# The order of work between the last attention chunk and the feed-forward: logits in two goes, the row softmax moved back, half rows side by side, slot weights in two halves

## The reference, cut to what matters

```python
# x: 3072 tokens x 320, from a gated recurrent attention over 4 batches x 8 heads x 768 steps x 40
logits = x @ phi                              # 3072 x 32: 8 experts with 4 slots each
d = softmax(logits, axis=0)                   # over tokens: what goes into a slot
slot_input = (d.T @ x).reshape(8, 4, 320)
slot_out[e] = relu(slot_input[e] @ w1[e]) @ w2[e]        # 320 -> 1024 -> 320
c = softmax(logits, axis=1)                   # over slots: how a token is put together
x = c @ slot_out.reshape(32, 320)
out = relu(x @ w_in) ** 2 @ w_out             # 320 -> 2048 -> 320
```

## Time and profile before

| | |
|---|---|
| median of 3 runs | 392.47 us (391.86 to 392.49) |
| profiled execution | 392.09 us |
| its span, first to last instruction | 390.4 us |
| PE busy in the span | 371.8 us (95%) |
| DVE, ACT, POOL busy | 236.3, 229.8, 81.9 us |
| granted TensorE clock | 1.00 throughout |

### The profile page before, as it was taken

How to read it: one execution, slowest core, us unless ns; L and a number is a source line. 1 busy time by engine, 2 the same in 40 slices (tenths; PEclk the granted TensorE clock), 3 DMA queues, 4 the chain that set the end, 5 groups by cost and what they waited for, 6 DMA issues and landing times.

```text
span 390.4 us, 9581 instructions
## 1 busy us (share of the span) xinstructions
PE 371.8 (95%) x3504; PEld 314.5 (81%) x3504; DVE 236.3 (61%) x556; ACT 229.8 (59%) x455; POOL 81.9 (21%) x122
## 2 busy tenths in 40 slices
PE   2899999989999999999999999999999999999996
PEld 2687777777677776345699999999999999999996
DVE  8767569558846954420487665565556556556553
ACT  3466667667576753021288666666666666666662
POOL 7276556455554730000000000000000000000000
PEclk9999999999999999999999999999999999999999
DMA  6499797787777769969100010010001001001001
GB/s 184 111 270 296 239 267 249 229 250 238 245 239 224 245 228 312 363 226 387 62 2 1 2 67 2 2 53 14 0 0 67 0 0 67 0 0 69 2 0 67
DMA packets 28392, 51.49 MB, mean 132 GB/s; under 512 B 2852, under 2 KB 19684, under 8 KB 28100
## 3 DMA queue, kind: packets, MB, share of 16 engines
q1 hardware_dynamic: 24884, 40.49, 33.3%
q10 hardware_dynamic: 3472, 10.51, 7.8%
HBM read 46.59 MB, written 4.33 MB: 130 GB/s over the span
## 4 chain that ended last, share of the span: by engine, by line
PE 89%; DVE 4%; ACT 2%; issue 2%; ACTq 1%; DMA 1%; POOL 0%; DVEq 0%
PE heads_banks L1119 7%; PE high_banks L1121 7%; PE high_banks L1120 7%; PE high_banks L1119 7%; PE heads_banks L1120 7%; PE heads_banks L1121 7%; PE low_banks L1107 6%; PE heads_banks L829 6%; PE low_banks L808 5%; PE heads_banks L822 3%; PE high_banks L844 3%; PE low_banks L788 3%; PE low_banks L861 3%; PE low_banks L1042 2%; PE high_banks L852 2%; PE low_banks L879 2%
## 5 line engine op out<-in xcount | busy, mean ns | idle before, releaser
L742 ACT ACTIVATE relu_h<-low_banks 128x512 f32<-128x512 f32 x96 | 57.5, 599 | 60.4 <-PE low_banks L1107 60.0
L1432 DVE CAST sq_hi<-sq_h 128x512 fp32r<-128x512 f32 x96 | 41.0, 427 | 66.7 <-ACT sq_h L747 66.1
L1434 DVE TENSOR_TENSOR sq_lo<-sq_h,sq_hi 128x512 fp32r<-128x512 f32 x96 | 66.5, 693 | 3.3
L747 ACT ACTIVATE sq_h<-relu_h 128x512 f32<-128x512 f32 x96 | 60.7, 632 | 3.1
L1120 PE MATMUL high_banks<-wo_lo,sq_hi 128*128 128x320 f32 x192 | 59.3, 309 | 0.0
L1121 PE MATMUL high_banks<-wo_hi,sq_lo 128*128 128x320 f32 x192 | 59.3, 309 | 0.0
L1119 PE MATMUL high_banks<-wo_hi,sq_hi 128*128 128x320 f32 x192 | 59.3, 309 | 0.0
L1119 PE MATMUL heads_banks<-wo_hi,sq_hi 128*128 128x320 f32 x192 | 59.3, 309 | 0.0
L1120 PE MATMUL heads_banks<-wo_lo,sq_hi 128*128 128x320 f32 x192 | 59.1, 308 | 0.0
L1121 PE MATMUL heads_banks<-wo_hi,sq_lo 128*128 128x320 f32 x192 | 59.0, 307 | 0.0
L1162 DVE TENSOR_TENSOR att_w<-low_banks,att_w 128x512 f32<-128x512 f32 x48 | 30.9, 685 | 31.5 <-PE low_banks L808 30.8
(11 more groups left out here) (181 smaller groups left out, 559.0 us busy)
## 6 DMA issues: line engine op xcount, KB each, us to landing
w_sb<-in_w SPq DMA_DIRECT2D x8, 1280.0 KB, 11.1
w_a<-in_w ACTq DMA_DIRECT2D x16, 512.0 KB, 5.4
kv_in<-in_kv SPq DMA_DIRECT2D x24, 320.0 KB, 4.0
qk_in<-in_qk SPq DMA_DIRECT2D x24, 256.0 KB, 3.3
o_in<-in_o_gate SPq DMA_DIRECT2D x24, 160.0 KB, 4.0
out<-out_sb SPq DMA_DIRECT2D x5, 640.0 KB, 3.2
wo_raw<-in_w_out SPq DMA_DIRECT2D x4, 640.0 KB, 11.5
w_b<-in_w ACTq DMA_DIRECT2D x8, 256.0 KB, 3.8
```

The costliest lines, as they stand in the source:

```text
L742: act.activation(relu_h[:, slot], bank[slot][:, :], ACT.Relu).then_inc(relu_done, 1)
L747: act.activation(sq_h[:, slot], relu_h[:, slot], ACT.Square).then_inc(sq_done, 1)
L1432: dve.tensor_copy(sq_hi[:, slot], sq_h[:, slot]).then_inc(hi_done, 1)
L1434: dve.tensor_tensor(sq_lo[:, slot], sq_h[:, slot], sq_hi[:, slot].bitcast(F32), ALU.subtract).then_inc(lo_done, 1)
```

## The change

1. **Logits in two goes.** The first two chunks of the last triple get their logits right behind the last `turn_heads`, the third alone after the last `turn_x`. Filler goes from 5 + 2 to 2 + 1.
2. **Row softmax behind the slots.** For the last batch `turn_logits` writes to bank 3, `turn_disp` does not wait for `row_relative` any more, and DVE runs `row_relative` after `slotsT`. `dispatch_exp` waits for the new maximum alone and comes ahead of `shrink`, `weigh_thirds` ahead of `row_exps`.
3. **Half rows side by side.** The 64 leftover rows of experts 0 to 3 lie in partitions 0 to 63 and those of experts 4 to 7 in 64 to 127, and likewise in `win_rest`; the matmuls on them are 64 rows deep, and the doubled and masked tiles are gone. `w1_b` and `win_rest` are loaded in this layout, `win_rest` with two DMAs.
4. **Order in the experts.** `expert_rest` is a function of its own, and the transposes of the first hidden half and one `turn_comb` lie between `expert_first(1)` and its second call, the other `turn_comb` behind it; both `turn_outs` come behind all of `expert_second`.
5. **Slot weights in two halves** of 1024 hidden columns, in banks 3 and 2, each with its own raise, lower, spread and copies; the first hidden tiles need the first half alone. The first hidden tile is squared and split in two halves as well (`first_tile`).

```diff
@@ 1, 2: PE and ACT after the last chunk
-            stay_awake(5)
-            turn_x(B - 1, NC - 1, 1)
-            stay_awake(2)
             pe.wait_ge(decay_exp, step_exps(B - 1, NC - 1))
-            logit(B - 1, NC - 1)
+            logit(B - 1, NC - 1, (0, 1))
+            stay_awake(2)
+            turn_x(B - 1, NC - 1, 1)
+            stay_awake(1)
+            logit(B - 1, NC - 1, (2,))
...
+                to = side_bank if rb < B - 1 else bank[3]
...
-                pe.wait_ge(row_chain, 7 * rb + 2)
+                if rb < B - 1:
+                    pe.wait_ge(row_chain, 7 * rb + 2)
...
-                act.wait_ge(max_chain, 4 * rb + 4)
+                act.wait_ge(max_chain, 4 * rb + 2)
...
-                act.activation(shrink[:, :], max_step[:, :], ACT.Exp).then_inc(shrink_ready, 1)
                 act.activation(disp_e[:, :, :], logitsT[:, :, :], ACT.Exp, bias=neg_new[:, 0:1],
                                accum_out=batch_sum[:, :]).then_inc(disp_ready, 1)
+                act.wait_ge(max_chain, 4 * rb + 3)
+                act.activation(shrink[:, :], max_step[:, :], ACT.Exp).then_inc(shrink_ready, 1)
@@ 3: half rows; the same in the fold, in turn_outs and for w_in
-                for g in range(2):
-                    for q in range(4):
-                        mm = pe.matmul(bank[2 * g + n][QUAD * q:QUAD * (q + 1), :], slotsT[:, 2 + n], w1_b[:, 4 * g + q],
+            def expert_rest(n):
+                for q in range(4):
+                    for g in range(2):
+                        rows = slice(DP * g, DP * (g + 1))
+                        mm = pe.matmul(bank[2 * g + n][QUAD * q:QUAD * (q + 1), :], slotsT[rows, 2], w1_b[rows, q, 512 * n:512 * (n + 1)],
                                        start=False, stop=True)
...
-            sp.dma_start(win_rest[:, :], w_in[2 * P:DM, :].rearrange("r (h n) -> (r h) n", h=2)).then_inc(win_loaded, 16)
+            quarters = w_in[2 * P:DM, :].rearrange("r (h u n) -> u r h n", h=2, u=2)
+            for u in range(2):
+                sp.dma_start(win_rest[DP * u:DP * (u + 1)], quarters[u]).then_inc(win_loaded, 16)
...
-                dve.scalar_tensor_tensor(out=slot_twice[:, :].rearrange("p (r h) -> p r h", h=2), in0=twice(slot_acc[:, plain:DM]),
...
-            keep_turned(slotsT, turned_bank).then_inc(slots_placed, 1)
+            dve.tensor_copy(slotsT[:, :, :], turned_bank[:, 0:KC * QUAD].rearrange("p (k s) -> p k s", k=KC)).then_inc(slots_placed, 1)
+            row_relative(B - 1)
@@ 5: slot weights and the first hidden tile, PE
+            def slot_weights(h):
+                for k in range(KC):
+                    for i in range(4) if k < 2 else (0, 2, 1, 3):
...
+                        mm = pe.matmul(bank[3 - h][QUAD * i:QUAD * (i + 1), 0:256], outsT[rows, k], cols, start=k == 0, stop=k == KC - 1)
+                mm.then_inc(sw_done, 1)
+            def spread_weights(h):
+                pe.wait_ge(sw_high, h + 1)
+                pe.wait_ge(sw_low, h + 1)
+                for i in range(4):
+                    rows = slice(QUAD * i, QUAD * (i + 1))
+                    if h == 1:
+                        pe.wait_ge(sw_ready[i % 2], i // 2 + 1)
...
@@ 5: ACT
+            high_weights(0)
+            high_weights(1)
+            copy_weights(0, 0)
+            copy_weights(0, 2)
...
+            def first_tile():
+                act.wait_ge(h_done, 1)
+                act.activation(relu_h[:, 0, 0:256], bank[0][:, 0:256], ACT.Relu).then_inc(half_relu, 1)
+                act.wait_ge(half_relu, 1)
+                act.activation(sq_h[:, 0, 0:256], relu_h[:, 0, 0:256], ACT.Square).then_inc(half_sq, 1)
+                copy_weights(1, 0)
+                copy_weights(1, 2)
+                act.activation(relu_h[:, 0, 256:512], bank[0][:, 256:512], ACT.Relu).then_inc(relu_done, 1)
+                act.wait_ge(relu_done, 1)
+                act.activation(sq_h[:, 0, 256:512], relu_h[:, 0, 256:512], ACT.Square).then_inc(sq_done, 1)
@@ 5: DVE
+            low_weights(0)
+            copy_weights(0, 1)
+            low_weights(1)
+            copy_weights(0, 3)
+            copy_weights(1, 1)
+            copy_weights(1, 3)
```

More of the change, by code:

```diff
@@ L294, in build_program @@
         expert_out = sem("expert_out")
-        expert_kept = sem("expert_kept")
+        expert_kept = [sem(f"expert_kept{i}") for i in range(2)]
         outs_turned = sem("outs_turned")
@@ L337, in half_of @@
             return (r + j) % 2
-        def twice(columns):
-            return columns.unsqueeze(2).broadcast_to([columns.shape[0], DM_LAST, 2])
         row_twice = row_rel[:, :, :].unsqueeze(2).broadcast_to([P, NC, 2, NS])
@@ L704, in _ @@
             act_step(B, 0, 0, nxt=False, cur=False)
-            for c in range(1, NC - 1):
+            for c in range(1, NC - 2):
                 act_step(B, c, 0, nxt=False, cur=False, prev=False, rb=B - 1)
@@ L868, in step_exps, with logit @@
                 return 2 * (step(b, c) + 3)
-            def logit(b, c):
-                pe.wait_ge(xT_ready, step(b, c) + 1)
+            def logit(b, c, thirds=range(TRI)):
+                pe.wait_ge(xT_ready, step(b, c) - 1 + thirds[-1])
                 pe.wait_ge(phi_loaded, 32)
@@ L877, in logit @@
                     rows = slice(0, min(P, DM - P * k))
-                    for q in range(TRI):
+                    for q in thirds:
                         mm = pe.matmul(logit_ps[QUAD * q:QUAD * (q + 1), :], phi_sb[rows, k], xT[rows, k, q], start=k == 0, stop=k == KC - 1)
-                mm.then_inc(logits, 1)
+                if TRI - 1 in thirds:
+                    mm.then_inc(logits, 1)
             def turn_logits(rb):
@@ L1047, in turn_outs @@
             def turn_outs(g):
-                pe.wait_ge(expert_kept, g + 1)
-                for k in range(KC + 1):
-                    mm = pe.matmul(bank[2][:, QUAD * k:QUAD * (k + 1)], outs_sb[:, g, P * min(k, 2):P * min(k + 1, 3)],
+                pe.wait_ge(expert_kept[g], 1)
+                for k in range(KC):
+                    width = P if k < 2 else DP
+                    mm = pe.matmul(bank[2][0:width, QUAD * k:QUAD * (k + 1)], outs_sb[:, g, P * k:P * k + width],
                                    fold_own[:, g], start=g == 0 and k == 0, stop=g == 1, skip_group_check=True)
+                mm = pe.matmul(bank[2][DP:P, 2 * QUAD:KC * QUAD], outs_sb[:, g, 2 * P:DM], fold_own[:, g],
+                               start=False, stop=g == 1, skip_group_check=True)
                 if g == 1:
@@ L1082, in _ @@
-            pe.wait_ge(win_loaded, 32)
-            for k in range(KC):
-                for i in range(4):
-                    part, cols = (outsT[:, k], win_sb[:, k, 512 * i:512 * (i + 1)]) if k < 2 else \
-                        (outsT[:, 2 + i // 2], win_rest[:, 512 * (i % 2):512 * (i % 2 + 1)])
-                    mm = pe.matmul(bank[3][QUAD * i:QUAD * (i + 1), :], part, cols, start=k == 0, stop=k == KC - 1)
-            mm.then_inc(sw_done, 1)
-            stay_awake(4, bank[0])
-            pe.wait_ge(spread_ready, 2)
@@ L1092, in _ @@
-            pe.wait_ge(sw_high, 1)
-            pe.wait_ge(sw_low, 1)
-            for i in range(4):
-                rows = slice(QUAD * i, QUAD * (i + 1))
-                for part in range(2):
-                    mm = pe.matmul(bank[4 + i][:, :], spread[rows, part].rearrange("p a b s -> p (a b s)"), sw_cols[rows, part],
-                                   start=part == 0, stop=part == 1)
-                mm.then_inc(sw_spread, 1)
+            def slot_weights(h):
+                for k in range(KC):
+                    for i in range(4) if k < 2 else (0, 2, 1, 3):
+                        rows = slice(0, P) if k < 2 else slice(DP * (i // 2), DP * (i // 2 + 1))
+                        cols = win_sb[:, k, sw_columns(h, i)] if k < 2 else win_rest[rows, h, 256 * (i % 2):256 * (i % 2 + 1)]
+                        mm = pe.matmul(bank[3 - h][QUAD * i:QUAD * (i + 1), 0:256], outsT[rows, k], cols, start=k == 0, stop=k == KC - 1)
+                mm.then_inc(sw_done, 1)
@@ new lines, in spread_weights @@
+            def spread_weights(h):
[5 more added lines that the diff above has]
+                        pe.wait_ge(sw_ready[i % 2], i // 2 + 1)
+                    for part in range(2):
+                        mm = pe.matmul(bank[4 + i][:, 256 * h:256 * (h + 1)], spread[rows, part].rearrange("p a b s -> p (a b s)"),
+                                       sw_cols[rows, part, 256 * h:256 * (h + 1)], start=part == 0, stop=part == 1)
+                    mm.then_inc(sw_spread, 1)
@@ L1112, in out_tile @@
                 slot = f % RING
-                pe.wait_ge(lo_done, NF * tb + f + 1)
+                halves = isinstance(tb, int) and (tb, f) == (0, 0)
+                if halves:
+                    pe.wait_ge(half_lo, 1)
+                else:
+                    pe.wait_ge(lo_done, NF * tb + f + 1)
                 for sub in range(NSUB):
```

(10 more changed lines are left out.)

133 lines of the change are left out of this document (74 added, 59 removed).

## The result

The changed kernel takes 387.01 us (386.70 to 387.61, 4 runs), the kernel before 392.48 us on the same chip: a ratio of 0.9863, interval 0.9847 to 0.9878. It is 5.5 us faster where 7.4 were forecast. The profiled execution took 386.7 us, its span is 385.0 us.

A forecast was written before the change was run, and what follows sets the result against it. The bound was taken as a chain of handoffs before a fixed-length feed-forward block on PE, so the second output tile's start decides. Savings 1.28 + 4.1 + 2.0 = 7.4 us gave 385.0 us, range 383.4 to 387.6.

The forecast's parts named there:

- DVE's wait for `wo_raw`: Ahead of the feed-forward: DVE waiting for this load was listed as a sign that the prediction is wrong.
- the attention phase at nothing: From the start to the last turn of the heads: forecast change 0.
- A: Chain up to the first expert matmul: 1.28 us sooner, from logits, dispatch turn, slots and fold.
- B: Experts, first expert matmul to first slot weight: 4.1 us shorter, 22.9 in place of 26.99 us.
- The half rows: The experts' two rests on leftover rows: 64-row tiles run eight at once, saving 1.4 us net of shape changes.
- the turns of `comb_parts` in the same shape: In the experts: these turns follow transposes in the same shape, saving about 0.2 us.
- the first wait for `hidT`: In the experts: covered by the second rest and the turns, with the fill of the weights, saving 0.6 us.
- The second wait: In the experts: the second wait for `hidT` is covered since `expert_second(1, 0)` comes first, saving 0.4 us.
- C: First slot weight to the feed-forward's second output tile: 2.0 us shorter, 9.4 in place of 11.38 us.
- the rival that the halves give nothing back: Slot weights to second output tile stays near 11.4 us, total 387.1; chance 0.2.
- The weights: Feed-forward loads: first `wo_raw` lands near 181.3, not 183.4; rival of over 1 us late, chance 0.06.
- The row softmax: Moved back behind the slots, its about 3.7 us of DVE and ACT work costs nothing.

The follow-up runs named there:

- e2: Kernel before with only the new form of the `w1_b` loads (64 partitions x 4 KB, on ACT); 393.03 us, ratio 1.0029.
- e3: Changed kernel with the `w1_b` loads back in the old form (128 partitions x 2 KB, on ACT); 386.46 us, ratio 0.9841.
- e1: Changed kernel with its eight `w1_b` loads issued by SP and not by ACT; 385.74 us, ratio 0.9837.
- e4: Changed kernel with one `w1_b` load for a pair of experts, four issues on ACT in place of eight; 386.15 us, ratio 0.984.
- e11: Changed kernel with the row softmax again ahead of the common maximum and the thirds' weights; 387.61 us, ratio 0.9876.
- e7: Changed kernel with the matmuls on the experts' leftover rows over 128 rows and not 64; 388.36 us, ratio 0.9905.
- e8: Changed kernel with slot weights, spread and first feed-forward tile on 512 columns in one go; 388.85 us, ratio 0.99.
- e9: e4 with the two `win_rest` loads issued by ACT behind its copies of the combine weights; 386.38 us, ratio 0.9836.
- e10: e9 with the fifth block of `wo` raised and lowered behind tile 1 of the feed-forward; 386.92 us, ratio 0.9841.

## Why the prediction was right, and where it was not

The forecast held in sign and, for the three stretches that it priced, in mechanism; the gain was 5.5 us and not 7.4. That 387.0 lies within the stated range of 383.4 to 387.6 is in part luck: it is outside the 384.2 to 386.3 that the forecast gave itself, and the range had been widened for rivals of which none cost anything in the changed kernel. One of the prediction's own signs of being wrong did appear, DVE's wait for `wo_raw`, though it cost nothing there.

- **The step that failed: the attention phase at nothing.** The prediction has no term for the loads into `w1_b`, whose new form holds ACT longer at each issue. The phase came 1.07 us later. e2 shows 0.83 of it from the form alone; e3, with the old form, has the three later steps gone (0.74). The other 0.24 has no shown cause. e1 and e4 gave 0.98 and 1.06 back, but they also take away what the old loads cost, so they show the place and not the size. The prediction had counted the added issue on SP's queue (0.45 us) and not the longer ones on ACT's.
- **A, -1.15 for -1.28.** The last logits gained 0.17 and not 0.43: they start 0.13 sooner and not 0.35, since the turn of x, behind two fillers, started 0.09 later and not 0.1 sooner. From their start to the kept logits 0.04 came back for 0.08. From the kept logits to the dispatch turn 0.55 came back for 0.48, which e11 confirms, and behind it 0.43 for 0.37.
- **B, -3.84 for -4.1.** The half rows gave what was said: 1.44 us by e7, which undoes them alone, for the 1.4 in the sum. A rest takes 1.02 for 1.83, and the 32 instructions on `w_a` ahead of it take 0.11 more (3.57 for 3.46, from start to start). What fell short is the order: the turns of `comb_parts` in the same shape and the first wait for `hidT` were priced at 0.2 and 0.6 and gave 0.51 together. The second wait and the second layer gave 0.46 for 0.4, and all from the first `turn_outs` on 1.47 for 1.5.
- **C, -1.88 for -2.0.** The second output tile does wait for ACT's square of tile 1, but 0.36 us and not 0.8, behind a first one that starts 0.2 later than said (190.53). The price of DVE compared unlike instructions (a copy of 256 columns out of PSUM, 0.42, with a subtraction on 512, 0.69), but the subtractions on 256 took 0.42 as well. e8 gives 1.84 us for the part by the medians and 2.00 by the marks, so the rival that the halves give nothing back, 387.1, was wrong, though its number is nearly the time that came: the same total from another cause.
- **The weights.** The landing was forecast near 181.3, at worst 182.7. It came at 183.81: `win_sb` was issued at 171.17 and not about 169.3, as the experts started 1.2 us later than forecast and took longer, and from there to the landing it took 12.6 us and not 12.0, while the loads into half of the partitions moved at 205 GB/s. Of the 2.5 us, 1.9 are thus the late issue. It cost nothing only since PE was late as well; e3, e9 and the profiled execution of e4 show the bill.
- **Behind the second tile** 0.26 us were lost evenly, 1.988 us for a tile and not 1.986. The same drift is in every run that is built on the changed kernel and not in e2, built on the kernel before. As e7, e8 and e11 have it too, neither the half rows of the experts' rests nor the halves of part 5 nor the late row softmax is its cause; no run looked for it further.
- **The row softmax** moved back cost nothing, as said: undoing it only loses.

## What to carry to other kernels

A transfer has two prices beside its bytes: the time that its issue holds the engine that issues it, and the rate at which its shape lets it move. Whoever halves the partitions of a load has to price both, on the issuing engine and for what is queued behind it. And a wait that ends 0.25 us before it costs anything caps the next gain; find it in the trace of the faster kernel, before more is built on it.

## What was unexpected in the hardware

- From the second pair on, issuing 512 KB on ACT's queue took 0.82 us as two loads of 128 partitions x 2 KB, 1.13 us as two of 64 x 4 KB and 0.63 to 0.65 us as one of 64 x 2 x 4 KB.
- A load whose outermost dimension was 2 kept an eighth of the DMA engines busy (share 0.13, 51 GB/s) and came over 8 us late. The Trainium skill, "SBUF — State Buffer", section "Can I just issue two DMAs to hit both halves?", says that two transfers to the two halves of the partitions gain next to nothing, and that issuing from several engines doesn't help either. The changed kernel agrees with the first, its two halves issued 0.6 us apart and 205 GB/s in all; e9, with both on ACT's queue beside SP's, agrees with the second (`wo_raw` at 184.04 against 184.12).
- The granted clock fell to half, for 3.4 us each time, 2.2 us behind the end of an idle stretch of PE of 0.66 us (e10) and 1.6 us behind one of 1.18 us (e4), and stayed at 1.00 behind one of 1.13 us (e9).
